# First chunk of an attention-to-experts kernel reordered: scores of batch 1, the last block of M and two state reads change places

## The reference, cut to what matters

```python
# B, H, S, Ns, D = 4, 8, 512, 32, 64
scores  = scale * x @ state.T            # softmax over the states
xread   = softmax(scores) @ state
scores2 = scale * state @ x.T            # softmax over the tokens
sread   = softmax(scores2) @ x
x = concat([xread, sread], axis=2)       # 4 * (512 + 32) rows of 512
h = x @ w_in                             # 512 -> 2048
g = h * tanh(softplus(h))                # mish
x = g @ w_out                            # 2048 -> 512
# then each row goes to one of 8 experts (argmax of a cosine logit)
out[rows of e] = gate * (relu(x @ w1[e]) @ w2[e])
```

## Time and profile before

| | |
|---|---|
| three executions | 746.26 us median (745.69 to 749.87) |
| the profiled execution | 742.25 us, its span 740.5 us |
| busy share of the span | PE 90%, PEld 69%, DVE 60%, ACT 52%, POOL 7% |
| granted PE clock, mean | 0.964 of full speed |

### The profile page before, as it was taken

One profiled execution on the slowest core, in us unless ns is written; L12 is line 12 of the kernel. 1 busy time (PEld: TensorE's weight loads), 2 busy tenths in 40 slices (PEclk: granted clock), 3 DMA queues, 4 the chain that ended last, 5 costly groups with the idle time before them and its releaser, 6 DMA issues.

```text
span 740.5 us, 12247 instructions
## 1 busy us (share of the span) xinstructions
PE 664.0 (90%) x4060; PEld 509.1 (69%) x4061; DVE 441.1 (60%) x671; ACT 385.2 (52%) x486; POOL 52.2 (7%) x75
## 2 busy tenths in 40 slices
PE   3538996999999999999989898399999999999995
PEld 1325774767876688666668686277888888888884
DVE  5685788676995869856577645463361262154261
ACT  2483676577775687666786534062342262253260
POOL 2000000000030000200000203001010101000001
PEclk9878999899999999999999999699999999999999
DMA  7622540630031300322300531373261162135140
GB/s 199 171 69 74 196 120 29 192 122 1 0 116 58 113 1 2 116 84 94 108 1 2 198 102 58 109 246 116 77 223 30 48 222 73 43 131 181 43 156 4
DMA packets 35221, 72.70 MB, mean 98 GB/s; under 512 B 5571, under 2 KB 5571, under 8 KB 35184
## 3 DMA queue, kind: packets, MB, share of 16 engines
q1 hardware_dynamic: 26640, 56.66, 24.1%
q0 software_dynamic: 3040, 9.13, 3.1%
q10 hardware_dynamic: 5504, 6.40, 3.1%
HBM read 60.92 MB, written 12.16 MB: 99 GB/s over the span
## 4 chain that ended last, share of the span: by engine, by line
PE 71%; DVE 13%; ACT 8%; issue 4%; DMA 3%; ACTq 1%; SPq 0%; POOL 0%; DVEq 0%; POOLq 0%
PE PS L639 16%; PE PS L661 16%; PE PS L545 15%; PE PS L513 8%; PE PS L465 3%; PE PS L478 2%; PE PS L648 2%; DVE ww L1228 2%; PE PS L438 2%; ACT ww L879 1%; ACT rr L875 1%; PE PS L604 1%; PE PS L620 1%; ACT ww L865 1%; ACT rr L873 1%
## 5 line engine op out<-in xcount | busy, mean ns | idle before, releaser
L545 PE MATMUL PS<-WH,gh 128*128 128x512 f32 x256 | 103.9, 406 | 0.0
L545 PE MATMUL PS<-WH,gl 128*128 128x512 f32 x256 | 101.2, 395 | 0.0
L545 PE MATMUL PS<-WL,gh 128*128 128x512 f32 x256 | 101.0, 394 | 0.0
L1223 DVE SCALAR_TENSOR_TENSOR qq<-ww,PS 128x1024 f32<-128x1024 f32 x34 | 41.3, 1215 | 65.4 <-ACT ww L867 65.3
L1322 DVE TENSOR_TENSOR WL<-raw,WH 128x1024 f32 (+1 forms) x48 | 57.0, 1221 | 37.9 <-ACT WH L940 37.8
L661 PE MATMUL PS<-WH,hh 128*128 (+1 forms) x168 | 68.6, 409 | 4.8 <-DVE hl L1332 4.8
L940 ACT ACTIVATE WH<-raw 128x1024 f32 (+1 forms) x48 | 48.7, 1056 | 36.1 <-issue 22.0
L661 PE MATMUL PS<-WH,hl 128*128 (+1 forms) x168 | 66.9, 398 | 0.0
L661 PE MATMUL PS<-WL,hh 128*128 (+1 forms) x168 | 66.5, 396 | 0.0
L865 ACT ACTIVATE ww<-PS 128x1024 f32<-128x1024 f32 x34 | 34.6, 1018 | 61.1 <-PE PS L513 57.9
L879 ACT ACTIVATE ww<-ww,cst 128x1024 f32<-128x1024 f32 x34 | 39.2, 1152 | 48.5 <-DVE ww L1228 48.5
(11 more groups left out here) (230 smaller groups left out, 1231.7 us busy)
## 6 DMA issues: line engine op xcount, KB each, us to landing
raw<-in_w SPq DMA_DIRECT2D x48, 512.0 KB, 4.4
raw<-in_w_in SPq DMA_DIRECT2D x40, 512.0 KB, 4.8
yg<-by_expert ACTq DMA_DIRECT2D x22, 260.0 KB
raw<-in_w_out SPq DMA_DIRECT2D x8, 512.0 KB, 3.9
by_expert<-junk SPq DMA_DIRECT2D x1, 2080.0 KB, 13.3
x_0a<-in_x SPq DMA_DIRECT2D x8, 128.0 KB, 5.8
x_0b<-in_x SPq DMA_DIRECT2D x8, 128.0 KB, 6.4
x_1a<-in_x SPq DMA_DIRECT2D x8, 128.0 KB, 6.6
```

Source lines behind the costliest of these rows:

```text
L545: mm = pe.matmul(PS[:, 2 + t, :], a[:, v % 2, e, t * P:t * P + P], w[:, 8 + p, e * 512:e * 512 + 512], start=(p == 0 and e == 0 and i == 0 ...
L1223: v.scalar_tensor_tensor(out=qq[:, u % 2], in0=ww[:, u % 2], scalar=4.0, in1=PS[:, bank:bank + 2, :], op0=ALU.subtract, op1=ALU.mult).then ...
```

## The change

In PE's order `score(1)` stays behind H(3) while `M(0, 3)`, `sread(0)` and `sread_turned(0)` each go back (behind H(4), H(5) and H(6)); `sread(1)` and `sread_turned(1)` go from behind Y(5) and Y(6) of chunk 0 to behind Y(3) and Y(4) of chunk 1. The split of the first g moves from unit 1 to the end of unit 0 on ACT and DVE. `exp_2`, `soft_5`, `M_hi`/`M_lo` of the last block, `sread_scale`, `soft_2(1)` and `soft_3(1)` move with them, and the waits are set anew. `r2` is doubled by parity of the batch, `E2D` of batch 1 gets a place of its own (over `Al`), and the turned read of batch 1 goes to bank 6.

```diff
@@ -155,7 +155,7 @@
         eT = sb_at("eT", [1, 2, E, NT], F32, stA_at)
         shn = sb("shn", [P, HG, D])
         r1 = sb("r1", [P, 3, HG * S // 32])
-        r2 = sb("r2", [P, 4, HG])
+        r2 = sb("r2", [P, 2, 4, HG])
         ident = sb("ident", [P, P])
         upper = sb("upper", [P, P])
         ones = sb("ones", [P, P])
@@ -202,7 +202,8 @@
         Al = sb_at("Al", [P, 2, HG, S], F32R, wl_at + 4 * SLOT)
         xT = sb_at("xT", [P, 2 * HG, S], F32, wl_at + 6 * SLOT)
         PT = sb_at("PT", [P, HG, S], F32, wl_at + 6 * SLOT)
-        E2D = [sb_at("E2D0", [P, HG, S], F32, wl_at + 5 * SLOT)] + [sb_at("E2D", [P, HG, S], F32, wl_at + 7 * SLOT)] * (B - 1)
+        E2D = ([sb_at("E2D0", [P, HG, S], F32, wl_at + 5 * SLOT), sb_at("E2D1", [P, HG, S], F32, wl_at + 4 * SLOT)]
+               + [sb_at("E2D", [P, HG, S], F32, wl_at + 7 * SLOT)] * (B - 2))
         gzh = sb_at("gzh", [P, 2, S], F32R, wh_at + 6 * SLOT)
         gzl = sb_at("gzl", [P, 2, S], F32R, wh_at + 7 * SLOT)
         gz = [sb_at("gz0", [P, 2, S], F32, wh_at + 4 * SLOT), sb_at("gz1", [P, 2, S], F32, wl_at + 4 * SLOT)]
@@ -431,7 +432,7 @@
             def score(b):
                 pe.wait_ge(st_d, 8 if b > 0 else 4)
                 if b > 0:
-                    pe.wait_ge(m_lo, NB * b)
+                    pe.wait_ge(m_lo, NB * b if b > 1 else 3)
                 for g in range(HG):
                     pe.wait_ge(x_tr, 4 * b + 2 * g + 2)
                     for d in range(2):
@@ -443,18 +444,17 @@
                 k = NB * c + nb
                 if k > 2:
                     pe.wait_ge(m_lo, k)
-                if c == 0 and nb == 2:
-                    pe.wait_ge(sc_e, 2)
+                if c == 0 and nb > 1:
+                    pe.wait_ge(sc_e, 2 * nb - 2)
                 if nb == 0 and c > 0:
                     pe.wait_ge(sc_e, 2 * c + 2)
-                if nb == 0 and c == 1:
-                    pe.wait_ge(shn_rdy, 2)
-                    pe.wait_ge(sh_e, 2)
+                if nb == 0 and c in (1, 2):
+                    pe.wait_ge(sh_e, 2 * c)
                 if nb == 0 and c > 1:
                     pe.wait_ge(idx_rdy, c - 1)
-                if nb == 1 and c > 0:
+                if nb == 1 and c > 1:
                     pe.wait_ge(shn_rdy, 2 * c + 2)
-                if nb == 2 and c > 0:
+                if nb == 2 and c > 1:
                     pe.wait_ge(sh_e, 2 * c + 2)
                 for g in range(HG):
                     r = RING["w", k, g]
@@ -468,10 +468,12 @@
 
             def sread(b):
                 pe.wait_ge(e2d_rdy, b + 1)
-                if b > 0:
+                if b > 1:
                     pe.wait_ge(m_lo, NB * b + 1)
+                elif b == 1:
+                    pe.wait_ge(rt_e, ST)
                 else:
-                    pe.wait_ge(sc_e, 4)
+                    pe.wait_ge(m_lo, NB)
                 for g in range(HG):
                     for t in range(16):
                         for j in range(4):
@@ -482,10 +484,10 @@
 
             def sread_turned(b):
                 pe.wait_ge(shn_rdy, 2 * b + 2)
-                if b > 0:
+                if b > 1:
                     pe.wait_ge(m_lo, NB * b + 2)
                 for g in range(HG):
-                    mm = pe.transpose(PS[0:D, 7, g * P:g * P + P], shn[:, g, :], ident[:])
+                    mm = pe.transpose(PS[0:D, 6 if b == 1 else 7, g * P:g * P + P], shn[:, g, :], ident[:])
                 mm.then_inc(sh_t, 1)
 
             pe.wait_ge(consts, 1)
@@ -677,13 +679,13 @@
                 if v + 2 < B * PC:
                     H(v + 2)
                 if c == 0:
-                    if p == 0:
-                        M(0, 3)
                     if p == 1:
                         score(1)
                     if p == 2:
+                        M(0, 3)
+                    if p == 3:
                         sread(0)
-                    if p == 3:
+                    if p == 4:
                         sread_turned(0)
                 if c in (1, 2):
                     if p == 1:
@@ -723,9 +725,13 @@
                 if c < 3:
                     if p == 0 and c > 0:
                         score(c + 1)
-                    if p == 5:
+                    if p == 3 and c == 1:
+                        sread(1)
+                    if p == 4 and c == 1:
+                        sread_turned(1)
+                    if p == 5 and c > 0:
                         sread(c + 1)
-                    if p == 6:
+                    if p == 6 and c > 0:
                         sread_turned(c + 1)
                     if p == 7:
                         M(c + 1, 3)
@@ -821,13 +827,13 @@
             def exp_2(b):
                 act.wait_ge(s2_m, b + 1)
                 for g in range(HG):
-                    a.activation(SC[:, g, :], SC[:, g, :], ACT.Exp, bias=r2[:, 1, g:g + 1], scale=1.0,
-                                 accum_out=r2[:, 2, g:g + 1]).then_inc(s2_x, 1)
+                    a.activation(SC[:, g, :], SC[:, g, :], ACT.Exp, bias=r2[:, b % 2, 1, g:g + 1], scale=1.0,
+                                 accum_out=r2[:, b % 2, 2, g:g + 1]).then_inc(s2_x, 1)
 
             def A_hi(b, gs=range(HG)):
                 act.wait_ge(af_rdy, HG * b + gs[-1] + 1)
-                if b == 1:
-                    act.wait_ge(sr_mm, 1)
+                if b == 1 or b == 2:
+                    act.wait_ge(sr_mm, b)
                 if b >= 2:
                     act.wait_ge(h_mm, (b - 1) * PC)
                 a.activation(Ah[:, b % 2, gs[0]:gs[-1] + 1], AF[:, gs[0]:gs[-1] + 1], ACT.Copy).then_inc(a_hi, len(gs))
@@ -835,7 +841,7 @@
             def sread_out(b):
                 act.wait_ge(sh_t, b + 1)
                 for h in range(2):
-                    ps = PS[0:D, 7, 0:HG * P].rearrange("p (g q r n) -> p g q r n", g=HG, q=2, r=2)
+                    ps = PS[0:D, 6 if b == 1 else 7, 0:HG * P].rearrange("p (g q r n) -> p g q r n", g=HG, q=2, r=2)
                     a.activation(sh[D * h:D * h + D, :, NS * b:NS * b + NS].rearrange("p (g q) n -> p g q n", g=HG), ps[:, :, :, h, :],
                                  ACT.Copy).then_inc(sh_e, 1)
 
@@ -963,7 +969,7 @@
                 n = p if kind == "m" else -1
                 done = c - 1 if kind == "m" else -1
                 mish_a(u)
-                if u >= 1 and SEQ[u - 1][0] == "m":
+                if u >= 2 and SEQ[u - 1][0] == "m":
                     mish_hi(u - 1)
                 if done >= 0:
                     if n == 3 and c < 3:
@@ -976,9 +982,14 @@
                     M_hi(c, n + 1)
                 if n == 7 and c < 3:
                     M_hi(c + 1, 0)
+                if c == 0 and n == 4:
+                    M_hi(0, 3)
                 if c == 0 and n == 5:
                     exp_1(1)
+                if c == 0 and n == 6:
                     sread_out(0)
+                if c == 1 and n == 6:
+                    sread_out(1)
                 if n == 4 and c in (1, 2):
                     exp_1(c + 1)
                 if n == 6 and c < 3:
@@ -1012,20 +1023,20 @@
                     if n > 0:
                         o_split(n)
                     if n == 0:
+                        mish_hi(0)
                         M_hi(0, 2)
+                    if n == 1:
                         exp_2(0)
-                    if n == 2:
-                        M_hi(0, 3)
                     if n == 3:
                         scores_out(1)
-                    if n == 5:
+                    if n == 6:
                         exp_2(1)
                 if c in (1, 2):
                     if n == 2:
                         scores_out(c + 1)
                     if n == 4:
                         exp_2(c + 1)
-                if kind == "m" and c > 0 and n == 0:
+                if kind == "m" and c > 1 and n == 0:
                     sread_out(c)
             mish_hi(LAST)
             load(t0)
@@ -1113,7 +1124,7 @@
             def turn_x(b, c):
                 for u in range(2):
                     dve.wait_ge(in_x[b][u], 64)
-                    if b > 1:
+                    if b > 2:
                         dve.wait_ge(sr_mm, b)
                     ins = v.transpose(xT[:, c, u * 256:u * 256 + 256].rearrange("p (t n) -> p t n", n=32),
                                       X2[b % 2][u][:, c // 2, :, 32 * (c % 2):32 * (c % 2) + 32])
@@ -1146,9 +1157,9 @@
                 v.tensor_tensor(pv, pv, of_token(0, gs).unsqueeze(2).to_broadcast([P, NW * len(gs), NS]), ALU.subtract).then_inc(p1_d, len(gs))
 
             def soft_2(b):
-                av_link(v.tensor_reduce(r2[:, 0, :], SC[:], AX, ALU.max))
+                av_link(v.tensor_reduce(r2[:, b % 2, 0, :], SC[:], AX, ALU.max))
                 av_join()
-                v.tensor_scalar(r2[:, 1, :], r2[:, 0, :], -1.0, None, ALU.mult).then_inc(s2_m, 1)
+                v.tensor_scalar(r2[:, b % 2, 1, :], r2[:, b % 2, 0, :], -1.0, None, ALU.mult).then_inc(s2_m, 1)
 
```

(28 more changed lines are left out.)

## The result

The changed kernel takes 751.03 us (median of 11 runs, 749.94 to 755.35); the kernel before, run beside it, 747.83 (11 runs, 744.62 to 750.27). The ratio is 1.0061, 95% interval 1.0035 to 1.0087: +4.6 us, where +6.0 was forecast. The medians alone lie 3.2 us apart: six executions of the changed kernel take 750 to 751 us and five 753 to 755. The ratio isn't that of the medians; it goes with the means, which lie 4.6 apart.

What follows compares the result with a forecast made beforehand. PE, busiest, was taken as the bound in chunk 1, with two earlier holes. Terms -3.4 + 5.0 + 3.1 + 1.3 = +6.0 us gave 748.2 on the profiled execution, 752.2 on the median; range 743 to 756.

Steps and rivals of the forecast that it cites:

- Part 1: First chunk, first g split at once: Y(0) begins at 50.6 instead of 61.5; H(2) 1.0 us later, at 46.0.
- "50 to 51": Sign that the forecast is right: the first L545 (Y) block begins at 50 to 51 us.
- Part 2: Scores of batch 1 ahead: PE waits 5.2 us for turned x, slow clock adds 1.8; Y(1) at 69.6.
- Part 3: M(0,3) and read of batch 0 later: transposes wait 2.4 us; Y(4) begins at 104.8, the lead used up.
- Part 4: Up to M(1,1): PE waits 6 us for its weights, half-rate block follows; Y(6) at 135.8, 3.4 us gained.
- Part 5: Read of batch 1 moved into chunk 1, where PE is the bound: costs 5.0 us.
- the slower rival: M(2,0)'s weights come over 2 us late behind load_x(3): +9 us, 755; chance 0.06.
- Part 6: Unit 14: sread_out(1) ahead of A_hi(2) on ACT delays e(14); the read of batch 2 waits 3.1 us more.
- the slow read: Read of batch 2 runs at the slow clock after its wait: 6.3 us for 5.0, 1.3 more.
- The faster one: Both first-chunk holes close and stay closed, Y(6) before about 126: -10 us, 736; chance 0.16.
- The "same" one: No stall at the read of batch 2, +1.6 us, 747.9; or PE's order does nothing, 746.3; chance 0.22.

Runs made afterwards that it cites:

- e8: e6 with the first g split in unit 1 again on ACT and DVE, exp_2(0) staying behind unit 1; 733.80 us, ratio 0.9788 to the kernel before.
- e3: Changed kernel with x of batch 1 turned on DVE at the end of unit 1 instead of unit 2; 745.93 us, ratio 0.9977 to the kernel before.
- e1: Changed kernel with sread_out(1) moved on ACT from ahead of A_hi(2) to behind unit 14's two exps; 747.42 us, ratio 0.9986 to the kernel before.
- e2: Changed kernel with M(1,1) moved on PE from ahead of Y(6) to behind it; 746.73 us, ratio 0.9975 to the kernel before.
- e5: Changed kernel with the read of batch 1 back in its old place, reordered first chunk kept; 740.72 us, ratio 0.9914 to the kernel before.
- e7: Kernel before the change with only the read of batch 1 moved to chunk 1, first chunk in old order; 755.72 us, ratio 1.0090.
- e4: Changed kernel with the edits of e1, e2 and e3 together; 734.64 us, ratio 0.9833 to the kernel before.
- e6: Changed kernel with the edits of e5 and e3 together; 733.57 us, ratio 0.9797 to the kernel before.

## Why the prediction was right

The forecast, 752.2 us, was +6.0; the timed runs say +4.6 by their ratio (median 751.03), the distance in the trace +5.6. By its steps:

- **Part 1** put the first L547 at 50.6 and H(2) at 46.0: 51.49 and 46.21. Counted from H(1), H(2) is 1.0 us later than before, as forecast; e8 shows that the early split costs 2.4 us there. H(2) itself was put at 4.5 us and took 5.3, all of it at half rate (46.21 to 51.49), so the first L547 came half a microsecond after the "50 to 51" that was to show it.
- **Part 2** put the scores at 64.4 behind a gap of 5.2, Y(1) at 69.6: 64.83, 4.66 and 70.01. e3 shows that this wait was worth 6.9 us to the end.
- **Part 3** put the new wait of the transposes at 104.5 and 2.4 us: 105.39 and 2.49. Not seen ahead: Y(4) behind it runs partly at half rate, 7.21 us to 112.76. It cost nothing, as H(8) waits for M_lo afterwards: 0.54 us here, 2.06 in e1, where Y(4) ran at full rate. The 1.4 us of `exp_1(1)` were right (1.39).
- **Part 4** put H(8) at 123.1 and Y(6) at 135.8: 123.82 and 135.22. The way there differs. I let the whole of M(1,1) wait and run at half rate; its first eight matmuls went ahead at 126.75, and only the other eight waited, until 133.29, 1.1 us later than forecast. They took 1.93 us where I had 3.64 for the whole block; that Y(6) starts within 0.6 us of the forecast is in part luck, as these two misses cancel. The price of the half rate was 2.0 us, where 1.8 was forecast: 1.0 in these eight and 0.96 in Y(6). Counted from H(1), Y(6) ends 3.2 us earlier than before (99.33 + 6.75 for 103.52 + 5.79), where 3.4 was forecast. e2 confirms that the DMA is what holds Y(6).
- **Part 5**: the read takes 5.35 us in chunk 1, where 5.0 was forecast. `load_x(3)` did not hold up M(2,0): that block starts at 214.00 with no idle time ahead of it, so the slower rival's mechanism was absent. The account is right as a difference to before, but its reading, that PE is the bound in chunk 1 and so the read costs 5.0, hid something. By e5 and e7 the read's old place was nearly free of cost, because PE would have waited there for M_lo and for the weights of M(1,1) anyway (e7, without the read there, ends Y(6) only 1.3 us sooner, counted from H(7)); the price belongs to the cover taken away, and part 4 should have booked it there.
- **Part 6** put e(14) at T + 4.2 and the wait at 3.4: T is 210.94, e(14) comes at 215.17, the wait is 3.27, 2.9 more than before. e1 removes it by moving one call.
- **The term that was mis-sized** is the slow read, "6.3 for 5.0: 1.3 more". The read of batch 2 took 5.40 us (224.99 to 230.39), 0.3 more than before (219.57 to 224.63). I had set the slow 6.34 against 5.0 without seeing that a microsecond of those 5.0 is a pause and no work (last section). Even the 0.3 isn't safe: in e1 the read at full rate took 5.42. The 6.34 stood behind a wait of 5.79, with the clock at 0.50 from its first matmul; behind the wait of 3.27 the clock fell only a microsecond into the read.

With the measured terms: -3.2 + 5.35 + 2.9 + 0.3 = +5.4, for +5.6 in the trace. The miss of the forecast against the timed runs, 1.4 us, is within what they leave open (+2.6 to +6.5).

**The rivals.** The faster one was to be decided by Y(6) before about 126; it came at 135.22. What was said against it, that `o_rest(7)` frees the weights late, is what e2 measures; whether the 3.2 us of waiting and moved work ahead of `o_rest(7)` are what makes it late was not tested by itself. The "same" one needed ACT and DVE to make up the stall of unit 14; they didn't. Its other form, that ACT and DVE set the pace whatever PE's order is, falls with e2, which changes PE's order alone and takes 6.2 us. As for the advice of the Trainium skill, page "TensorE: Matmul & The Clock Gate", section "HAM oscillation", to leave PE no idle stretches: e4 and e6 show what following it is worth here (1.7% and 2.0%), and the change shows that filling two holes isn't following it as long as what released them stays late: the idle time up to H(16) only moved, 24.8 before and 26.5 after, while e6 really takes it out, 14.7.

**A version that beats both.** e6: the scores ahead of M(0,3), x turned a unit earlier, the read of batch 1 where it was. 733.57 us (median of four executions) beside 748.80, ratio 0.9797 (0.9742 to 0.9853).

## What to carry to other kernels

Before moving work out of a place next to a hole, ask what lands, copies or drains under it there: the read stood where the weights of the next block were in flight, and its move cost more (10.3 us on the reordered chunk, 7.4 on the old one) than the read's own 5.4. On an engine that works in order, a short instruction that waits for another engine belongs behind the work of its unit, not ahead of it: 0.56 us of copying held up ACT by 3.2. And take a change of several parts apart as soon as its sum is near nothing: here the reordering was worth -4.8 us and the move of the read +10.3, and a single move of `turn_x` gained 6.9 (e3).

## What the runs showed of the hardware that I had not expected

**The clock can fall after the work has come back.** The stretches around the read of batch 2 in the changed kernel (length, busy time of PE, PEld, DVE, ACT, POOL, then PEclk, DMA share and GB/s):

```profile
221.00:223.00 2.00, 0.71 (x4) 0.23 (x2) 2.00 (x3) 1.97 (x3) 0.00 (x0) 1.00 0.10 37
223.00:225.00 2.00, 0.01 (x3) 0.04 (x4) 2.00 (x3) 0.57 (x1) 0.00 (x0) 1.00 0.00 0
225.00:227.00 2.00, 2.00 (x112) 2.00 (x116) 2.00 (x2) 0.99 (x1) 0.00 (x0) 0.76 0.00 0
227.00:229.00 2.00, 2.00 (x85) 2.00 (x81) 1.33 (x2) 0.15 (x1) 0.00 (x0) 0.50 0.03 8
229.00:230.00 1.00, 1.00 (x67) 1.00 (x61) 0.00 (x0) 0.00 (x0) 0.00 (x0) 0.78 0.00 0
```

PE stood from about 221.7 to 225 at the full grant, 2.4 GHz, and fell to 0.50, the 1.2 GHz level, when it was at work again, until about 229.5. It isn't always so. In the longer waits of the same kernel the clock fell while PE still stood: ahead of the scores it was at 0.50 from 63 us on (they start at 64.83), and ahead of the second half of M(1,1), at 133.29, the stretches show

```profile
128.00:130.00 2.00, 0.00 (x0) 0.00 (x0) 1.97 (x4) 1.97 (x3) 0.00 (x0) 1.00 0.00 0
130.00:132.00 2.00, 0.00 (x0) 0.00 (x0) 2.00 (x3) 0.47 (x1) 0.00 (x0) 0.61 0.81 218
```

A shorter wait, 2.49 us ahead of the transposes, was followed by 0.50 from 107 to 109.9, in Y(4), too; one of 2.30 at the same place in e1 was not. The price beyond the wait was 2.15 us in the scores (5.18 for 3.03), 2.0 in M(1,1) and Y(6) and 0.3 in the read, though the read ran at 0.50 for about 3.5 us.

**A read at full rate has a pause of its own.** In the 256 small matmuls PE stops once with no other engine named: 1.37 us in the chain above, 1.00 to 1.66 in the full-rate reads of all the traces up to 230 us. A read that starts behind a long wait and runs mostly at half rate shows none: that of batch 1 before (6.34 us), those of batch 2 in the changed kernel, e2, e3 and e7 (5.40 in all four). The one at 88.72 in e7 lies between: a pause of 2.14, and half rate behind it. By these parts the slow read cost so little: 4.06 us of matmuls and a pause of 1.00 before, 5.40 without a pause after. What makes the pause was not tried. It can cost more than itself: in e8 it was 1.66 us, with PE idle for 0.36 ahead of the read, and the H behind it took 4.55 us where it takes 2.95 elsewhere. Its chain, and its windows:

```profile
206.82 3.21 PE PS L477 x212
210.03 1.66 issue
211.69 0.86 PE PS L477 x44
212.55 4.55 PE PS L512 x12
```

```profile
212.00:213.00 1.00, 1.00 (x39) 0.86 (x29) 0.41 (x2) 0.00 (x0) 0.00 (x0) 1.00 0.08 16
213.00:214.00 1.00, 1.00 (x4) 0.77 (x4) 0.06 (x1) 0.00 (x0) 0.00 (x0) 0.57 0.00 0
214.00:216.00 2.00, 2.00 (x7) 1.54 (x6) 0.00 (x0) 0.00 (x0) 0.00 (x0) 0.50 0.00 0
```

In e6, with a pause of 1.01 us at the same place, that H took 2.94. That such differences are why executions of one kernel differ by some us is a guess; it was not tested.
